# First expert weights loaded as sixteen half experts, three rows to a partition, in place of twenty-four row blocks

## The reference

```python
# stage 1, for each step t
cur = einsum(u * k_t, v_t)
y_t = einsum(r_t, state + cur)
state = w * state + einsum(k_t, v_t)
# stage 2: x is 3072 x 384, phi 384 x 32, w1[e] 384 x 1024, w2[e] 1024 x 384
logits = x @ phi
d = softmax over tokens of logits
slot_input = (d.T @ x).reshape(8, 4, 384)
h = maximum(slot_input[e] @ w1[e], 0); slot_out[e] = h @ w2[e]
x = (softmax over slots of logits) @ slot_out
# stage 3
h = x @ w_in                  # 384 x 2048
return (h * sigmoid(1.702 * h)) @ w_out
```

## Time and profile before

| | us |
|---|---|
| median of 3 runs | 389.57 |
| lowest and highest run | 388.96, 389.83 |
| the profiled execution | 389.61 |
| its span, first to last instruction | 387.8 |
| PE busy | 375.5 (97%) |
| DVE, ACT, POOL busy | 229.2, 187.4, 111.7 |

### The profile page before, as it was taken

How to read it: one execution, slowest core, us unless ns; L and a number is a source line. 1 busy time by engine, 2 the same in 40 slices (tenths; PEclk the granted TensorE clock), 3 DMA queues, 4 the chain that set the end, 5 groups by cost and what they waited for, 6 DMA issues and landing times.

```text
span 387.8 us, 9112 instructions
## 1 busy us (share of the span) xinstructions
PE 375.5 (97%) x3224; PEld 296.0 (76%) x3224; DVE 229.2 (59%) x419; ACT 187.4 (48%) x432; POOL 111.7 (29%) x125
## 2 busy tenths in 40 slices
PE   7889899999999999899999999999999999999996
PEld 6778687877876344578888888888888888888885
DVE  6787778787774301286665565555556655655560
ACT  1235454545444431576655546454655465455552
POOL 5987798887682020144400000000000000000000
PEclk9899999999999999999999999999999999999999
DMA  7999999999999999900002001000200020002002
GB/s 232 289 315 394 382 355 405 403 370 358 402 336 370 328 334 403 378 26 3 0 0 84 0 0 67 16 0 0 81 0 0 0 81 0 0 0 81 0 2 82
DMA packets 28966, 63.77 MB, mean 164 GB/s; under 512 B 3088, under 2 KB 17056, under 8 KB 28560
## 3 DMA queue, kind: packets, MB, share of 16 engines
q1 hardware_dynamic: 27600, 62.99, 44.6%
q10 hardware_dynamic: 1344, 0.49, 0.7%
HBM read 58.75 MB, written 4.72 MB: 164 GB/s over the span
## 4 chain that ended last, share of the span: by engine, by line
PE 79%; DMA 7%; POOL 6%; issue 3%; DVE 2%; SPq 2%; ACT 0%; DVEq 0%; POOLq 0%
PE bank L598 11%; PE bank L597 11%; PE bank L596 11%; PE pair L596 6%; PE pair L598 5%; PE pair L597 5%; PE bank L341 5%; PE pair L380 4%; DMA ring<-win 4%; PE bank L583 4%; DMA krb<-kr 3%; PE pair L371 3%; PE pair L363 3%; PE bank L401 2%; POOL rkn L1046 2%
## 5 line engine op out<-in xcount | busy, mean ns | idle before, releaser
L825 DVE TENSOR_TENSOR gf<-bank,sg 128x512 f32<-128x512 f32 x72 | 49.7, 692 | 63.4 <-ACT sg L993 63.1
L993 ACT ACTIVATE sg<-bank 128x512 f32<-128x512 f32 x72 | 42.9, 598 | 73.3 <-PE bank L583 73.2
L597 PE MATMUL bank<-ghi,whi 128*128 128x512 f32 x192 | 74.7, 389 | 0.0
L596 PE MATMUL bank<-glo,whi 128*128 128x512 f32 x192 | 74.7, 389 | 0.0
L598 PE MATMUL bank<-ghi,wlo 128*128 128x512 f32 x192 | 74.7, 389 | 0.0
L831 DVE TENSOR_TENSOR glo<-gf,ghi 128x512 fp32r<-128x512 f32 x96 | 69.4, 723 | 0.2
L999 ACT ACTIVATE ghi<-gf 128x512 fp32r<-128x512 f32 x96 | 60.0, 625 | 0.9 <-DVE gf L825 0.8
L873 ACT ACTIVATE yt<-pair 112x512 f32<-112x512 f32 x24 | 14.3, 598 | 57.7 <-PE pair L380 57.7
L596 PEld LDWEIGHTS bank<-glo,whi 128*128 128x128 f32 x192 | 36.0, 188 | 7.5
L597 PEld LDWEIGHTS bank<-ghi,whi 128*128 128x128 f32 x192 | 36.0, 188 | 7.5
L598 PEld LDWEIGHTS bank<-ghi,wlo 128*128 128x128 f32 x192 | 36.0, 188 | 7.5
(11 more groups left out here) (162 smaller groups left out, 535.0 us busy)
## 6 DMA issues: line engine op xcount, KB each, us to landing
ring<-w SPq DMA_DIRECT2D x24, 512.0 KB, 6.3
rkb<-rk SPq DMA_DIRECT2D x23, 512.0 KB, 5.4
krb<-kr SPq DMA_DIRECT2D x24, 384.0 KB, 5.6
ring<-w SPq DMA_DIRECT2D x4, 1536.0 KB, 14.5
ring<-w SPq DMA_DIRECT2D x8, 768.0 KB, 10.4
vb<-v SPq DMA_DIRECT2D x24, 192.0 KB, 5.6
out<-ob SPq DMA_DIRECT2D x18, 256.0 KB, 2.1
ring<-win SPq DMA_DIRECT2D x3, 1024.0 KB, 14.1
```

What stands on the lines that cost most here:

```text
L596: pe.matmul(o, w_hi, lo, start=(f == 0), stop=False)
L597: pe.matmul(o, w_hi, hi, start=False, stop=False)
L825: dve.tensor_tensor(gf[:, f % 2, :], bank[f % 4][:, :], sg[:, f % 2, :], ALU.mult).then_inc(gf_ok, 1)
L993: act.activation(sg[:, f % 2, :], bank[f % 4][:, :], ACT.Sigmoid, scale=1.702).then_inc(sg_ok, 1)
```

## The change

The matrix w1 of an expert is laid out with rows 3p, 3p+1 and 3p+2 on partition p, which are 12288 neighbouring bytes in memory. An expert is loaded in two halves of 6144 bytes to a partition (768 KB each, 16 in all). Chunks 1 to 4 issue one half in each of the first three steps and none in the fourth; chunk 5 issues one in each of its four steps. For this SP's loop covers two chunks in one pass, so that three halves of the first chunk and three of the second make three experts. Since the k-th third of a slot now holds the rows 3p + k, the three matmuls for `snt` take every third column of `acc` in place of blocks of 128.

```diff
+PIECE = SLOT_W // 2
...
-        w1_v = w1.rearrange("e (k p) f -> (e k) p f", p=P)
+        w1_v = w1.rearrange("e (p k) f -> e p (k f)", p=P)
...
-            def step(c, b):
+            def step(c, b, e0=0, x=0):
...
-                if not is_first(c):
-                    for i in (b,) if b < B - 1 or is_last(c) else (b, b + 1):
-                        piece = (B + 1) * (c - 1) + i
-                        sp.dma_start(ring_flat[:, bass.ds(piece * FE, FE)], w1_v[piece]).then_inc(w1_in, 16)
+
+                if not is_first(c) and (b < B - 1 or is_last(c)):
+                    e, half = e0 + (x + b) // 2, (x + b) % 2
+                    sp.dma_start(ring_flat[:, bass.ds(e * SLOT_W + half * PIECE, PIECE)],
+                                 w1_v[e][:, half * PIECE:(half + 1) * PIECE]).then_inc(w1_in, 16)
...
-            steps(sp, step)
+            for b in range(B):
+                step(0, b)
+            with sp.Fori(0, (C - 2) // 2) as g:
+                for c in range(2):
+                    for b in range(B):
+                        step(2 * g + c + 1, b, 3 * g, 3 * c)
+            for b in range(B):
+                step(C - 1, b, E - 2)
...
-                last = pe.matmul(YN[:, 32 * m:32 * m + 32], acc[:, m * P:(m + 1) * P], samef[:, :],
+                last = pe.matmul(YN[:, 32 * m:32 * m + 32], acc[:, m:DM:KD], samef[:, :],
                                  start=True, stop=True)
...
-            pe.wait_ge(w1_in, 16 * KD * E)
+            pe.wait_ge(w1_in, 16 * 2 * E)
```

## The result

The changed kernel takes 393.44 us as the median of four runs (391.0 to 396.4), against 389.7 us before (388.96 to 389.85): a ratio of 1.0103, 95% interval 1.0071 to 1.0135. Seven more runs in the experiments gave 392.88 us, ratio 1.0086 (1.0054 to 1.0117). Predicted were 392.8 us, within 389.6 to 394.3. The profiled execution took 392.93 us with a span of 391.1 us, 3.3 us more than before. The time thus came out near the sum, but several of its terms did not, as the rows show; part of the agreement is luck.

A forecast was written before the change was run, and what follows sets the result against it. The prediction took the landing of step 7's krb to set the end, PE's later waits being paid in full. To 389.61 us it added 1.9 + 0.1 + 1.2 = 3.2 us, giving 392.8 us, range 389.6 to 394.3.

The forecast's parts named there:

- (1): Chunk 1: larger w1 pieces ahead of step 7's krb make PE start step 8 later, 1.9 us (1.7 to 2.3).
- Rival C: Steps 5 to 7: each extra 256 KB hides under a fixed w1 transfer cost; 389.7 us, chance 0.11.
- my 338 GB/s by landings: Steps 5 to 7: rate from two steps' 1.64 MB each in 9.7 us between krb landings; gave 2.3 us as upper end.
- (2): Fourth step of chunks 1 to 4: issuing no w1 piece there costs nothing and gains nothing, zero.
- (3): Chunk 5: loading 3072 KB of w1 in place of 2048 costs zero, with less ahead of its krb transfers.
- (4): snt matmuls: every third acc column as stationary operand slows six weight loads, 0.1 us taken, 0 to 1.15 us.
- (5): SP: 16 issues in place of 24 and a loop body twice as long, zero.
- (6): PE's clock: a wait of about 2.6 us ahead of step 8 brings a fall to 0.50, 1.2 us.
- rival A: Step 8: the later landing without a fall of the clock; 391.6 us, chance 0.27.
- B: Steps 5 to 8: krb's short rows pass w1's long ones, so krb lands earlier; 388.4 us, chance 0.10.

The follow-up runs named there:

- l0: Kernel before with SP's steps written out, three neighbouring rows to a partition and strided columns of acc, old order and 512 KB pieces: 390.04 us, ratio 1.0024.
- b1: Kernel before with SP's steps written out and w1 begun one step later: 389.38 us, ratio 1.0016.
- u0: Changed kernel with SP's 24 steps written out in place of its loop, same transfer order and sizes; a control: 392.28 us, ratio 1.0062.
- u1: As u0, but the w1 half of step 22 goes with step 19: 392.62 us, ratio 1.0072.
- u3: As u0, but chunk 5's third half goes behind the inputs of step 23: 392.1 us, ratio 1.0073.
- v1: As u0, but rk padded with 16 zero rows so the last rkb moves 128 partitions, not 112: 391.28 us, ratio 1.0051.
- s1: Kernel before, own layout, SP's steps written out, its 512 KB pieces spread as nearly as possible in the change's order: 392.94 us, ratio 1.0099.
- v2: Kernel before with only the last rkb made 128 partitions in place of 112: 389.13 us, ratio 0.9991.
- h1: Changed kernel's 768 KB halves and strided columns, SP's steps written out, order near the kernel before's: 390.34 us, ratio 1.002.

## Why the prediction was right, and where it was not

**What bounds.** Right in the main: from step 8 on each wait of PE is paid in full. Step 8 is one such place; the end of chunk 5 is a second that I held to be covered. But that the landing of the `krb` of step 7 sets the end of the kernel was read from one execution, whose wait of 1.18 us l0 and b1 do not have.

**(1), the larger pieces in chunk 1: 1.9 us predicted.** Over the seven profiles with the new order in chunk 1 (the change twice, u0, u1, u3, v1 and s1) steps 5 to 8 take 14.65 to 15.99 us, 15.4 on average, and over the five with the old or nearly the old one (before, l0, v2, h1, b1) 13.47 to 14.72, 13.8. That is 1.6 us. The size holds against this average; against the profile that I counted from, 14.72 us, it is 0.7. The way there was told wrongly: I had a full queue add 0.65 us at each of three steps. POOL's waits for `krb` at steps 5, 6 and 7:

```profile
30.58 1.00 POOL L1050 TENSOR_TENSOR rkn<-krb 128x384 f32<-128x384 f32 x1 [1.90 <-DMA krb<-kr]
...
35.24 1.01 POOL L1050 TENSOR_TENSOR rkn<-krb 128x384 f32<-128x384 f32 x1 [0.83 <-DMA krb<-kr]
...
40.41 1.00 POOL L1050 TENSOR_TENSOR rkn<-krb 128x384 f32<-128x384 f32 x1 [1.34 <-DMA krb<-kr]
```

The delay comes with the first of them: that `krb` is on its way for 6.5 us in place of 5.9, and POOL waits 1.90 us in place of 0.96. The landings of steps 5 and 7 are then 9.8 us apart, as before (9.7 us), though 3712 KB were issued between them in place of 3200. Rival C foresaw this, but not for its reason. The queue had no room. The windows over that time, first of the kernel before, then of the changed one (columns as in the earlier trace rows):

```profile
28.00:32.00 4.00, 4.00 (x92) 3.49 (x84) 2.50 (x6) 1.92 (x7) 2.96 (x4) 1.00 1.03 393
32.00:36.00 4.00, 4.00 (x72) 3.34 (x70) 2.88 (x6) 2.28 (x10) 2.75 (x4) 1.00 1.03 404
36.00:40.00 4.00, 4.00 (x72) 2.84 (x71) 3.23 (x6) 2.01 (x10) 3.00 (x5) 1.00 1.04 400
```

```profile
28.00:32.00 4.00, 4.00 (x88) 3.32 (x88) 2.50 (x4) 1.40 (x6) 2.02 (x3) 1.00 1.04 416
32.00:36.00 4.00, 4.00 (x87) 3.27 (x76) 3.23 (x8) 1.44 (x8) 3.17 (x4) 1.00 1.03 406
36.00:40.00 4.00, 4.00 (x66) 3.37 (x64) 3.11 (x7) 2.17 (x9) 2.99 (x4) 1.00 1.02 385
```

From landing to landing (29.03 to 38.78 us before, 30.58 to 40.41 after) both kernels moved 395 GB/s, 3.9 MB, which in the kernel before is 0.6 MB more than was issued between the two transfers. So my 338 GB/s by landings was no rate of the queue: when a transfer lands, part of the next ones has been moved already. The first piece of w1 behind that `krb`, 512 KB issued at 33.33 us, landed 5.8 us later, only 0.4 us after it. What sets the distance is a loop. SP may issue that `krb` only after POOL's `kk` of step 5, 3.2 us after the `krb` of step 5 landed, in both kernels, and it is then 6.5 or 6.6 us on its way. The late landing at step 5 thus moves the issue as well: it comes 4.8 us after that of the w1 half of step 6, in place of 3.7. At 400 GB/s 1.1 us more are some 440 KB, by this estimate more than the 256 KB by which that half is larger.

**(2), no piece in the fourth step:** right, no gain, and in the changed kernel chunks 2 to 4 keep their 18.64 us.

**(3), chunk 5, is the step that failed:** zero predicted, and 1.15, 0.70 and 1.14 us measured in the two profiles of the change and in u0, 1.0 on average. I counted from the fourth step of chunk 4, where 256 KB less are ahead of the `krb` of step 23, and took a lighter sum for a shorter queue. In the last three steps alone 2304 KB of w1 are issued ahead of it in place of 1536. And I did not see that the windows around 110 us were slow in the trace of the kernel before.

**(4), the strided columns:** 0.1 us taken, 0.38 measured. The rule of the Trainium skill ("SBUF — State Buffer", cachelines), that each element of a new line costs, was borne out in direction: 262 ns a load in place of 192, a third more and not twice. The upper end of 1.15 us, which by that rule was the nearer one, was not.

**(5), fewer issues:** zero was taken; u0's interval meets the change's, so nothing else is shown.

**(6), the clock:** such falls occur, but the wait of 2.6 us that was to bring one did not, and their share was mis-sized. A fall costs 1.54 us, where I had taken 1.2 out of at most 1.6. But it came in three of seven executions, after waits of 1.3 to 1.6 us, and so costs about 0.7 us on average. In the first profile of the change it did not come, and there rival A's account of step 8 holds. It may explain part of the spread of the change's 11 runs: the four with a mean clock of 0.991 or less took 394.0 us on average, the other seven 392.7.

**The sum.** 1.6 + 0.7 + 1.0 + 0.38 = 3.7 us by the profiles, 3.7 and 3.5 us by the two sets of runs, 3.2 predicted. Errors of opposite sign, 0.8 us too much in (1) and (6) and 1.3 us too little in (3) and (4), made the forecast look better than its steps were. The sum leaves out the time before step 5, which varies by up to 2 us from one profile to another. Rival A lacked (3); B did not occur; of C the landings of steps 5 to 7 came true, neither its reason nor its time.

## What to carry to other kernels

Where small inputs and large prefetches share one queue, count what stands ahead of each input when it is issued, step by step, and not only the total: the same 12 MB in another order cost up to 1%, and rows half as long again cost nothing that could be told. A load moved a step earlier only moved the wait here (u1). Bytes issued between two landings are not the bytes that were moved: take the rate from the windows, and look for a loop that sets the distance. And take a wait that exists in one profile for the property of a kernel only after a second profile. A transfer of 112 partitions among ones of 128 deserves a look at GB/s against the DMA share.

## What the runs showed that I had not expected

Near the one `rkb` of 112 partitions the DMA engines were over 1.00 busy while moving 221 to 278 GB/s in the changed kernel and 244 to 315 before, for some 4 us; with 128 partitions at the same place they moved 398 to 424 GB/s. Its rows may be dealt out to the engines in another way than those of the other transfers; no run here shows that.

Rows of 6144 bytes gained and cost nothing that could be seen (h1 against l0: 1.002 and 1.0024).
